# Attention in groups of four heads of two batches, with wider loads, a one-operation value sum and single root steps

## What is computed

```python
B, H, S, D = 4, 8, 576, 64          # batches, heads, positions, head size
# 1. attention over positions averaged in fours (144 of them), repeated back to 576
out_d = softmax(q_d @ k_d.T / 8) @ v_d           # q_d, k_d, v_d: means over 4 positions
# 2. attention over the band |i - j| < 4
out_local = softmax(where(band, q @ k.T / 8, -1e9)) @ v
x = repeat(out_d, 4) + out_local                  # then 2304 tokens of 512 values
# 3. x / rms(x) * rms_g, a gated layer 512 -> 1536 -> 512
y = (silu(xn @ w_gate) * (xn @ w_val)) @ w_out
# 4. a layer 512 -> 2048 -> 512 with the square of relu
out = relu(y @ w_in) ** 2 @ w_out2
```

## Time and profile before

| | us |
|---|---|
| median of 3 runs | 1044.17 |
| lowest and highest run | 1040.68, 1045.19 |
| profiled execution, its own time | 1042.85 |
| span of its trace | 1041.1 |
| DMA moved | 42.85 MB |

### The profile page before, as it was taken

One profiled execution on the slowest core, in us unless ns is written; L12 is line 12 of the kernel. 1 busy time (PEld: TensorE's weight loads), 2 busy tenths in 40 slices (PEclk: granted clock), 3 DMA queues, 4 the chain that ended last, 5 costly groups with the idle time before them and its releaser, 6 DMA issues.

```text
span 1041.1 us, 16089 instructions
## 1 busy us (share of the span) xinstructions
PE 994.5 (96%) x6404; PEld 923.4 (89%) x6404; DVE 425.5 (41%) x783; ACT 314.2 (30%) x650; POOL 188.2 (18%) x175
## 2 busy tenths in 40 slices
PE   5888669999999999999999999999999999999998
PEld 4666557999999999999999998999999999999997
DVE  5748975453353343443442322323333233232322
ACT  3435434433212212212222433322322222222221
POOL 5467764761000000000000662000000000000000
PEclk9968877899999999999999999999999999999999
DMA  9997511340000000000000431000000000000000
GB/s 187 190 173 149 105 48 31 109 125 1 1 1 1 1 1 1 1 1 1 1 1 31 122 124 49 1 1 31 1 31 1 1 31 1 1 31 1 31 1 31
DMA packets 22447, 42.85 MB, mean 41 GB/s; under 512 B 2150, under 2 KB 5222, under 8 KB 21798
## 3 DMA queue, kind: packets, MB, share of 16 engines
q1 hardware_dynamic: 20742, 40.64, 16.0%
q10 hardware_dynamic: 1632, 1.18, 0.5%
HBM read 37.10 MB, written 4.72 MB: 40 GB/s over the span
## 4 chain that ended last, share of the span: by engine, by line
PE 91%; DVE 4%; issue 2%; ACT 1%; DMA 1%; POOL 1%; SPq 0%; DVEq 0%; ACTq 0%; POOLq 0%
PE bank L948 48%; PE bank L1047 19%; PE bank L979 15%; PE bank L925 2%; PE bank L886 2%; PE bank L900 2%; PE bank L880 1%; PE bank L904 1%; PE bank L935 1%; DMA kp<-k_dram 1%; DVE vd L691 1%; PE bank L875 1%; PE bank L851 0%; DVE xT L729 0%; DVE sml L678 0%
## 5 line engine op out<-in xcount | busy, mean ns | idle before, releaser
L948 PE MATMUL bank<-xs,wsplitB 128*128 128x384 f32 x2376 | 436.8, 335 | 0.0
L948 PEld LDWEIGHTS bank<-xs,wsplitB 128*128 128x128 f32 x2376 | 416.7, 188 | 6.9
L1047 PE MATMUL bank<-wsplitB 128*128 128x512 f32 x702 | 174.4, 393 | 0.0
L1047 PEld LDWEIGHTS bank<-wsplitB 128*128 128x128 f32 x702 | 130.7, 188 | 23.7
L806 DVE TENSOR_TENSOR prod<-sig 128x384 f32<-128x384 f32 x96 | 53.6, 558 | 222.2 <-ACT sig L602 222.2
L979 PE MATMUL bank<-hb,wsplitB 128*128 128x384 f32 x720 | 136.0, 336 | 1.4 <-ACT hb L539 1.4
L979 PEld LDWEIGHTS bank<-hb,wsplitB 128*128 128x128 f32 x720 | 125.7, 188 | 3.0 <-POOL wsplitB L425 1.6
L764 DVE TENSOR_TENSOR prod<-prod,bank 128x384 f32<-128x384 f32 x72 | 39.9, 554 | 191.6 <-PE bank L948 191.5
L602 ACT ACTIVATE sig<-bank 128x384 f32<-128x384 f32 x96 | 47.2, 492 | 229.6 <-PE bank L948 229.6
L539 ACT CAST hb<-prod 128x384 fp32r<-128x384 f32 x72 | 37.0, 514 | 253.9 <-DVE prod L764 253.9
L948 PE MATMUL bank<-xs,wsplitA 128*128 128x384 f32 x504 | 95.3, 340 | 0.0
(11 more groups left out here) (77 smaller groups left out, 768.8 us busy)
## 6 DMA issues: line engine op xcount, KB each, us to landing
wrawB<-w_dram SPq DMA_DIRECT2D x56, 256.0 KB, 3.0
vquad<-v_dram SPq DMA_DIRECT2D x4, 1152.0 KB
out_dram<-work SPq DMA_DIRECT2D x18, 256.0 KB, 2.0
kp<-k_dram SPq DMA_DIRECT2D x6, 576.0 KB, 20.6
qs<-q_dram SPq DMA_DIRECT2D x6, 576.0 KB, 23.7
vwin<-v_dram SPq DMA_DIRECT2D x3, 1024.0 KB
wrawA<-w_dram SPq DMA_DIRECT2D x12, 256.0 KB, 8.1
vwin<-v_dram SPq DMA_DIRECT2D x1, 640.0 KB
```

Of the source, the lines that this page charges most:

```text
L948: last = mm(bank[:, 0:cols], wslot(n)[:, pw, 128 * k:128 * k + 128], x[:, px, k, 0:cols], start=(i == 0 and k == 0), stop=(i == 2 and k == ...
L1047: last = mm(OUT[par][tt][:, :], gs[:, px, 128 * tt:128 * tt + 128], w[:, pw, :], start=(m == 0 and i == 0), stop=(m == J2 - 1 and i == 2))
```

## The change

The four batches become four groups: group b holds heads 4*(b % 2) to 4*(b % 2) + 3 of the two batches 2*(b // 2) and the next, one batch on each half of the partitions. A local unit has 64 queries of four heads of both batches, a downsampled unit one pair of heads of one batch, whose score products both read the same half of the partitions and write different halves.

- Loads of k and q are one transfer of 128 partitions each. The value windows come by batch with rows of 1 KB (twice the transfers), `vquad` as 128 and 16 partitions by batch, and the 144 value sums lie on 128 + 16 partitions, so that a downsampled value product sums over 128 and then over 16 rows.
- `sum_values` is one reduction over four positions, for the 128 partitions at i = 10 and for the 16 at i = 12, both with 2048 inputs to a partition.
- Downsampled units have no `subtract`: ACT makes the negated scaled maximum (`mul`), and then three exponentials straight from PSUM with it as bias. PE may write the bank again once they are done (exp_done).
- DVE runs `maxima(g)`, `subtract(g)`, and then `sums(g - 1)`, where it ran the sums first.
- POOL's `sum_four` stands at i = 1, 2, 3, 4, 7, 8 (in the first group as before), `add_down` at 5, 6, 11, 12.
- The sums of squares move to 35, 36, 38 and `mean_square` to 38, the 12 root steps to one a unit from 39 to 50, and `normalise` and the splits of the first tokens behind the last unit; PE runs the last units' products before and after the gate product in another order.

```diff
-ROOT_AT = (34, 37, 40, 42)
-NORM_AT = (43, 45)
-SPLIT_X_AT = (46, 49)
-SUM_FOUR_AT = (3, 4, 5, 6, 7, 8)
-SUM_V_AT = (10, 11, 12)
-ADD_DOWN_AT = (9, 10, 11, 12)
+SQUARES_AT = (33, 34, 36)
+SUM_SQ_AT = (35, 36, 38)
+MEAN_SQ_AT = 38
+ROOT_AT = tuple(range(39, 51))
+NORM_AT = (51, G_ALL)
+SPLIT_X_AT = (G_ALL, G_ALL)
+SUM_FOUR_AT = (1, 2, 3, 4, 7, 8)
+FIRST_SUM_FOUR_AT = (3, 4, 5, 6, 7, 8)
+SUM_V_AT = (10, 12)
+ADD_DOWN_AT = (5, 6, 11, 12)
+ADD_DOWN_OF = (0, 2, 1, 3)
...
             def load_vquad(b):
-                ready(sp, vd_done, 3 * b)
-                sp.dma_start(vquad[:, :, :, :],
-                             v_d[b].rearrange("(a p r) n -> p a r n", a=2, r=FACTOR)).then_inc(vq_in, 16)
+                ready(sp, vd_done, 2 * b)
+                for x in range(2):
+                    v = v_d[batch0(b) + x][:, D * head0(b):D * head0(b) + GC].rearrange("(p r) n -> p r n", r=FACTOR)
+                    sp.dma_start(vquad[0][:, x, :, :], v[0:HK[0], :, :]).then_inc(vq_in, 16)
+                    sp.dma_start(vquad[1][:, x, :, :], v[HK[0]:SD, :, :]).then_inc(vq_in, 16)
+            def rows_of(src, b, t0, t1):
+                return src[batch0(b):batch0(b) + 2, :, head0(b):head0(b) + NH, t0:t1].rearrange("b d h s -> (b d) h s")
             def load_k(b, t0, t1, done):
-                for h in range(2):
-                    sp.dma_start(kp[b % 2][64 * h:64 * h + 64, :, HALO + t0:HALO + t1],
-                                 k_d[b, :, h::2, t0:t1]).then_inc(done, 16)
+                sp.dma_start(kp[b % 2][:, :, HALO + t0:HALO + t1], rows_of(k_d, b, t0, t1)).then_inc(done, 16)
...
             def exponent(g):
-                act.wait_ge(sub_done, g + 1)
-                scale = SCALE if local(g) else SCALE / FACTOR ** 2
-                nc.scalar.activation(weights_of(g), weights_of(g), ACT.Exp, scale=scale).then_inc(exp_done, 1)
+                w = weights_of(g)
+                if local(g):
+                    act.wait_ge(sub_done, nth(g) + 1)
+                    nc.scalar.activation(w, w, ACT.Exp, scale=SCALE).then_inc(exp_done, 1)
+                else:
+                    n, scale = nth(g), SCALE / FACTOR ** 2
+                    act.wait_ge(mx_done, g + 1)
+                    nc.scalar.mul(nmd[:, n % DRING], maxima_of(g), -scale).then_inc(nm_done, 1)
+                    ...
+                    for x in range(NQ):
+                        last = nc.scalar.activation(w[:, x, :], scores_of(g)[:, x, :], ACT.Exp,
+                                                    bias=nmd[:, n % DRING, x:x + 1], scale=scale)
+                    last.then_inc(exp_done, 1)
...
-            def sum_values(b, n):
-                ...
-                nc.vector.tensor_tensor(vd[:, :, :], first, vquad[:, :, n + 1, :], ALU.add).then_inc(vd_done, 1)
+            def sum_values(b, half):
+                dve.wait_ge(vq_in, 64 * (b + 1))
+                ready(dve, pv_done, NU * b)
+                nc.vector.reduce_sum(vd[half][:, :, :], vquad[half][:, :, :, :].rearrange("p b r n -> p b n r"),
+                                     AX).then_inc(vd_done, 1)
...
             for g in range(G_ALL):
-                b, i = batch_of(g), g % NU
+                b, i = group_of(g), g % NU
+                maxima(g)
+                if local(g):
+                    subtract(g)
                 if g > 0:
                     sums(g - 1)
-                maxima(g)
-                subtract(g)
                 if i in SUM_V_AT:
                     sum_values(b, SUM_V_AT.index(i))
                 if g in SUM_SQ_AT:
                     sum_squares(0, (SUM_SQ_AT.index(g),))
                 if g in ROOT_AT:
-                    root(0, ROOT_AT.index(g))
-                ...
+                    root_step(0, ROOT_AT.index(g))
             sums(G_ALL - 1)
+            dve.wait_ge(misc_in, 16)
+            for half in range(2):
+                normalise(0, half)
+                split_x_low(0, 0, half)
...
                 else:
-                    p = i - NL
+                    p, x = down(g)
                     for a in range(NQ):
-                        for rows in halves:
-                            last = mm(bank[rows, SD * a:SD * a + SD], qd[rows, p, QD * a:QD * a + 64],
-                                      kd[rows, p, :], start=True, stop=True, skip_group_check=True)
+                        for h in range(2):
+                            last = mm(bank[halves[h], SD * a:SD * a + SD],
+                                      qd[halves[x], 2 * p + h, QD * a:QD * a + 64],
+                                      kd[halves[x], 2 * p + h, :], start=True, stop=True, skip_group_check=True)
...
-            pe.wait_ge(sub_done, G_ALL - 2)
-            gate(0, 0, 0)
             transposes(G_ALL - 3)
             values(G_ALL - 4)
             transposes(G_ALL - 2)
             values(G_ALL - 3)
-            pe.wait_ge(sub_done, G_ALL)
-            value(0, 0, 0)
+            pe.wait_ge(exp_done, G_ALL - 2)
+            gate(0, 0, 0)
             transposes(G_ALL - 1)
             values(G_ALL - 2)
+            pe.wait_ge(exp_done, G_ALL)
+            value(0, 0, 0)
             values(G_ALL - 1)
```

340 lines of the change are left out of this document (178 added, 162 removed).

## The result

The changed kernel takes 1054.52 us (median of 4 runs, 1050.77 to 1060.05) where the kernel before, run beside it, takes 1042.84 (1040.68 to 1045.19). The ratio is 1.0125, 95% interval 1.0094 to 1.0155: slower by 1.25%. I had said 1042, within 0.5%, and a range to 1054, and the time lies half a microsecond over that range. The profiled execution has a time of its own of 1050.77 and a span of 1048.8, so it is the lowest of the four and its trace shows nearly 4 us less than the median. Executions that took over 1.5% longer than the fastest of their kernel count in the medians given here, but not in the ratios.

A forecast was written before the change was run, and what follows sets the result against it. Only the first 183 us could move, with DVE and PE nearly even at full clock, PE deciding at half clock, DVE and POOL at batch ends. Stage terms summed to -1.0 from 1042.85, so 1041.8, said as 1042; range 1030 to 1054.

The forecast's parts named there:

- Start: PE's start of unit 2, from 11.97 to 9.0 us by wide k and q loads: gain 3.0, bounds 0 and 4.
- To unit 13: Unit 13's start from 41.78 to 36.4: load wait 1.1 and DVE 2.5 saved, 1.2 lost to POOL's later q sum.
- To unit 26: Unit 26's start from 83.0 to 77.6: PE's pace at half clock unchanged, no gain or loss, bounds -9 and +1.5.
- Rival 1: Second group's long half-clock stretch from 60 us doesn't return, the gap before it perhaps shorter: 1032 us, chance 0.25.
- To unit 35: Unit 35's start from 107.65 to 101.6: POOL binds, stage of 24.0 us, gain 0.6, bounds -2 and +1.5.
- To the value products: Unit 35's value products, 124.25 to 123.1: PE waits at `mean_square` for DVE, stage 21.5 us, loss 4.9, bounds 2.5 and 8.
- To unit 48: Unit 48's start from 152.98 to 146.9: lighter DVE, 23.8 us for 28.7, gain 4.9, bounds -8 and +1.5.
- Rival 2: The wait at `mean_square` behind unit 38 holds PE's clock at 0.50 up to unit 48: +10, 1052 us, chance 0.22.
- To `gate`: `gate` from 168.15 to 167.9: scaling, cast, subtraction now ahead of it, 21.0 us for 15.2, loss 5.8, bounds 3 and 8.
- Rival 3: The value reduction takes twice as long for its stride, 4.6 us each, mostly on the path: 1055 us, chance 0.07.
- signs that I had named for a wrong prediction: Start unmoved, reduction over 3.5 us, or PE's clock by stretch more than 15 us of half clock from today's.

The follow-up runs named there:

- experiment 7: The changed kernel with each wide load of k and q issued as two transfers of 64 partitions: 1054.55 us, ratio 1.0109.
- experiment 4: The changed kernel with 14 unread products on PE ahead of its wait for POOL's q sum in each group: 1050.12 us, ratio 1.0078.
- experiment 2: The changed kernel with its value reduction reading adjacent elements, without the 1 KB step (values wrong): 1057.63 us, one time taken.
- experiment 8: The kernel before with DVE's sums of unit g - 1 behind the maxima and subtraction of unit g: 1045.54 us, ratio 1.0009.
- all of the repairs: The change with POOL's q sums earlier, mean square later, root steps, scalings and splits inside the loop: 1037.12 us, ratio 0.9946.

## Why the prediction was wrong

*Start* (predicted 9.0, 10.54). Direction right, size off: 1.4 us for my 3.0. The ratio of 1.6 that I read out of the earlier trace rows was too high; the same stretch moves 239 GB/s now for 197, and by experiment 7 the width makes 239 for 204 and 2.5 us of start. With halves unit 2 starts 1.1 us later than before (13.05), near the 1 us that I had for the other loads. The trace agrees in direction with what the Trainium skill says of 64 partitions and half of the ports (SBUF — State Buffer, Door 1: The DMA port swizzle), with 1.21 for its 2, and 1.17 by experiment 7.

*To unit 13* (36.4, 42.37): **the step that failed.** I had seen that POOL's last sum of q ends later, and put 1.2 us on it, but I gave no price to the clock behind the wait: units 9 to 12 at 1.2 GHz, 3.69 us apart for 2.06. The wait of 3.38 itself isn't the loss, for unit 9 starts 17.4 us behind unit 2 where before it was 18.2 and my terms made 19.4. From unit 9 to unit 13 it takes 14.39 us, for 11.60 before and 8.0 by my terms (less 1.1 and 2.5); with the clock held it is 8.48 (experiment 4). So the term that I put at nothing is 5.9 us. (The saving that I wrote as 2.5 is 2.3 by its own figures, 12 less 9.7.) In the kernel before units 10 and 11 start 2.06 apart (32.91 and 34.97) in spite of a gap of 2.94 at 26.91, and I took full clock for what this group has. POOL runs from 14.94 to 27.9 us without a pause, so behind 14.94 faster loads and a lighter DVE only bring PE earlier to a sum that doesn't come earlier; only an earlier start of that chain moves it (experiment 7).

*To unit 26* (-3.3 against my zero). The stretch from 60 us still has half clock, 16.9 us behind the POOL wait where before has at least 22.7 (60.0 to 82.7), and the gap of 2.94 us at 57.05 is gone, like the one at 26.91. Rival 1 named both; it had the gap right and the clock wrong, since the wait for POOL took the gap's place, as I had held against it.

*To unit 35.* POOL binds, as predicted, 25.2 us for my 24.0. Its chain of sums starts 6.2 us behind unit 26 (86.53) for my 4.4, since the last normalisation of `pd` (0.91) and a wait of 1.12 for DVE's sums come first; it then runs 19.0 us without a pause, for my 20.2.

*To the value products* (23.8 us for 21.5, inside my bounds). The wait at `mean_square` is there, 5.41 us, ended by DVE's last sum of squares, as the prediction has it. DVE between units 35 and 38:

```profile
112.22 3.72 DVE L724 TENSOR_REDUCE vd<-vquad 128x512 f32<-128x2048 f32 x1
...
119.59 3.59 DVE L724 TENSOR_REDUCE vd<-vquad 16x512 f32<-16x2048 f32 x1
123.12 0.54 DVE L732 TENSOR_TENSOR work<-work 128x384 f32<-128x384 f32 x1
```

The product starts 18.2 us behind unit 35 for my 0.9 + 14.0. About 1.6 of the 3.3 is again the clock: PE is at 0.50 all the way to unit 38, the case for which I had 15.6 and not 14.0. Some 1.4 is the second reduction; experiment 2, with 2.26 us for it, starts the product 1.3 us sooner. The first is hidden, as DVE waits 0.70 us for PE once more before unit 38's maximum (118.35). The reduction takes the same for 16 partitions as for 128. What lies behind the product took 1.0 us less than I had.

*To unit 48* (22.0 for 23.8). Near. Rival 2, in which the clock stays at 0.50 from that wait to unit 48, didn't happen in the profiled execution: it is 1.00 from 128.0 to 148.5.

*To `gate`* (25.2 us for 21.0, over my upper bound of 15.2 + 8 = 23.2): **the second step that failed.** I had put this stage between half and full clock; it is at half clock from one end to the other, for which I had 23. In front of `gate` DVE runs the chain that I had named:

```profile
165.35 3.70 DVE L724 TENSOR_REDUCE vd<-vquad 16x512 f32<-16x2048 f32 x1
...
169.69 1.80 DVE L769 SCALAR_TENSOR_TENSOR xT<-xT,gvec,work 128x384 f32<-128x384 f32 x2
172.44 0.96 DVE L775 TENSOR_TENSOR xs<-xT,xs 128x768 fp32r<-128x768 f32 x1 [0.95 <-ACT xs L545]
173.31 1.14 DVE L769 SCALAR_TENSOR_TENSOR xT<-xT,gvec,work 128x384 f32<-128x384 f32 x2
175.41 0.96 DVE L775 TENSOR_TENSOR xs<-xT,xs 128x768 fp32r<-128x768 f32 x1 [0.95 <-ACT xs L545]
```

6.8 us from the first scaling to `gate`, for my 5.9: the first pair of scalings takes 0.90 each, partly beside POOL's last normalisation of `pd`, the second 0.57. Ahead of it maximum, sums and reduction take 5.6 us behind unit 51's scores for my 4.3, and that is the reduction. So of the 4.2 us over my 21.0 the clock has 2.0, the reduction 1.4 and the chain 0.9.

*Rival 3*, the reduction twice as long for its stride, is instructive. Its size came true (3.68, over the 3.5 from which it should decide), and its total too, 1055 for 1054.5, yet its mechanism came true in small part: it put 14 us on the path, and with the reduction at 2.26 the starts of stages give back some 2.8 (experiment 2). At half clock PE's own pace hides the rest. The Trainium skill's rule that stands behind it is that each access that crosses to a new 16-byte line pays a penalty (SBUF — State Buffer, Door 1: The DMA port swizzle). Experiment 2 agrees with it, with the factor 1.63. A total that fits doesn't prove a rival.

So: the waits at units 35 and 48, at `mean_square`, `gate` and `project` were in the prediction, with place and cause; of the two new ones, that at unit 9 stood there as 1.2 us of lateness, and that at unit 22 (3.16 us) only as an argument against rival 1. What failed is the clock behind them: nothing in the first group, a value between the two levels in the third and fourth, where the trace has 0.50 throughout. Two of the signs that I had named for a wrong prediction came: a reduction of over 3.5 us, and over 15 us more at half clock (96 for 72 in the first 200 us). That the time lies only half a microsecond over the range is no merit: the range ended there for rival 2, which didn't happen.

## What to carry to other kernels

Where PE's clock drops behind its waits, price a wait on PE with the half clock of the work behind it: in the first group here a wait of 3.4 us was followed by 5.9 us of lost pace. Compare the half clock of whole executions and not the number of waits, since a wait can also take the place of a gap that was there before (experiment 8). When DMA and DVE get lighter, look first at the engine whose sum stands next in PE's way (POOL's here) and at the order of its list; two entries moved by two units were worth 1.1%, all of the repairs 1.8%. And take a suspected price out for itself before it is blamed: the reduction was 60% dearer than reckoned, eight times 1.4 us, and of these 11 us only some 2.8 were on the path.
